# End of attention in an attention + two-MoE kernel: own PSUM banks for the last group, a softplus without reciprocal, first expert weights split between groups

## What is computed

```python
# 1. attention: each token is a mix of itself and its 6 predecessors, per head
w = softmax(weight_gen, axis=-1)                     # (B, S, 8 heads, 7 taps)
out = einsum('bshk,bskhg->bshg', w, x_unfolded)      # x_unfolded: 7 shifted rows
# 2. first mixture of experts (8 experts, 2 choices a token)
logits = x @ w_gate
noise_scale = log1p(exp(x @ w_noise))                # softplus
noisy = logits + noise_scale * noise
top2, top2_w = two largest of noisy, softmax over the two
out[mask] += top2_w * (relu(x[mask] @ w1[e]) @ w2[e])
# 3. second mixture (8 experts, 1 choice), by cosine to expert_emb over tau
logits = normalized(x) @ normalized(expert_emb).T / tau
out[mask] = gate_w * (relu(x[mask] @ w1[e]) @ w2[e])
```

## Time and profile before

| | us |
|---|---|
| median of 3 runs (1231.30, 1233.33, 1233.25) | 1233.25 |
| the profiled execution | 1230.78 |
| its span, first to last instruction | 1229.0 |
| outside the span | 1.78 |
| attention, up to the end of the last row sum | 120.2 |
| logits of the last group copied | 126.6 |
| first mixture's PE stream begins | 206.4 |

### The profile page before, as it was taken

How to read it: one execution, slowest core, us unless ns; L and a number is a source line. 1 busy time by engine, 2 the same in 40 slices (tenths; PEclk the granted TensorE clock), 3 DMA queues, 4 the chain that set the end, 5 groups by cost and what they waited for, 6 DMA issues and landing times.

```text
span 1229.0 us, 27241 instructions
## 1 busy us (share of the span) xinstructions
PE 1098.7 (89%) x8062; PEld 1041.1 (85%) x8062; DVE 753.6 (61%) x1412; ACT 548.3 (45%) x1543; POOL 523.5 (43%) x635
## 2 busy tenths in 40 slices
PE   1999168999999999999999999787289999999997
PEld 0566056999999999999999999766279999999997
DVE  8998896546465554646545464476854654466663
ACT  2112266445454544545445454356644554455552
POOL 5878102444444444444444444400324444444444
PEclk9999589999999999999999999989589999999999
DMA  9111200313122131312213111173712313124511
GB/s 330 67 58 65 60 1 21 95 42 95 38 73 67 41 102 42 94 38 79 64 41 97 39 37 38 40 257 104 239 50 72 100 39 102 40 61 128 141 56 36
DMA packets 51188, 97.89 MB, mean 80 GB/s; under 512 B 9651, under 2 KB 33051, under 8 KB 50876
## 3 DMA queue, kind: packets, MB, share of 16 engines
q1 hardware_dynamic: 33084, 61.77, 16.4%
q0 software_dynamic: 18048, 35.42, 9.9%
HBM read 69.62 MB, written 29.10 MB: 80 GB/s over the span
## 4 chain that ended last, share of the span: by engine, by line
PE 78%; DVE 13%; issue 3%; POOL 2%; ACT 2%; DMA 2%; DVEq 0%; POOLq 0%; ACTq 0%; SPq 0%
PE banks L605 22%; PE banks L607 11%; PE banks L591 9%; PE banks L597 7%; PE banks L596 7%; PE banks L592 7%; PE banks L593 7%; DVE prods L856 3%; PE banks L567 2%; POOL prods L415 2%; PE banks L575 2%; PE banks L576 2%; PE banks L529 1%; DVE choices L1064 1%; PE banks L519 1%
## 5 line engine op out<-in xcount | busy, mean ns | idle before, releaser
L1014 DVE SCALAR_TENSOR_TENSOR h_lo<-banks,h_hi 128x256 fp32r<-128x256 f32 x736 | 312.0, 424 | 373.6 <-ACT h_hi L743 319.0
L743 ACT ACTIVATE h_hi<-banks 128x256 fp32r<-128x256 f32 x736 | 282.5, 384 | 450.8 <-PE banks L597 340.1
L605 PE MATMUL banks<-w_hl,h_hi 128*128 128x384 f32 x1472 | 466.4, 353 | 0.0
L607 PE MATMUL banks<-w_hl,h_lo 128*128 128x192 f32 x1472 | 371.1, 252 | 0.0
L607 PEld LDWEIGHTS banks<-w_hl,h_lo 128*128 128x128 f32 x1472 | 279.6, 190 | 0.0
L605 PEld LDWEIGHTS banks<-w_hl,h_hi 128*128 128x128 f32 x1472 | 276.0, 188 | 0.2
L430 POOL DMA_INDIRECT x_slots<-token_rows,gather_idx x192 | 192.3, 1002 | 107.2 <-POOL gather_idx L427 76.8
L591 PE MATMUL banks<-x_hi_a,w_hi 128*128 (+1 forms) x736 | 224.9, 306 | 1.7 <-DVE x_hl_b L982 1.7
L592 PE MATMUL banks<-x_hi_a,w_lo 128*128 (+1 forms) x736 | 206.6, 281 | 0.0
L597 PE MATMUL banks<-x_hl_b,w_lo 128*128 (+1 forms) x736 | 206.3, 280 | 0.0
L596 PE MATMUL banks<-x_hl_b,w_hi 128*128 (+1 forms) x736 | 205.8, 280 | 0.0
(11 more groups left out here) (172 smaller groups left out, 1271.7 us busy)
## 6 DMA issues: line engine op xcount, KB each, us to landing
raw<-in_moe_w SPq DMA_DIRECT2D x17, 768.0 KB
choices<-choice_rows SPq DMA_DIRECT2D x28, 384.0 KB, 3.8
raw<-in_moe_w SPq DMA_DIRECT2D x17, 512.0 KB
raw<-in_moe_w SPq DMA_DIRECT2D x34, 256.0 KB
x_halo<-in_x SPq DMA_DIRECT2D x2, 2688.0 KB, 15.0
token_rows<-stage SPq DMA_DIRECT2D x14, 384.0 KB, 2.3
token_rows<-rows SPq DMA_DIRECT2D x14, 384.0 KB, 3.9
x_slots<-token_rows,gather_idx POOLq DMA_INDIRECT x192
```

Source lines behind the costliest of these rows:

```text
L605: mm(y[:, i, 0:2 * D], h_hi[:, c % HBUFS, t], w2_hl[u][:, c, :, :], start=c == 0, stop=False)
L607: ins = mm(y[:, i, 0:D], h_lo[:, c % HBUFS, t], w2_hl[u][:, c, 0, :], start=False, stop=c == FC - 1)
L743: sc.activation(h_hi[:, c % HBUFS, :], banks[:, c % HBANKS, 0:BLOCK], ACT.Relu).then_inc(h_hi_ready[m], 1)
L1014: v.scalar_tensor_tensor(h_lo[:, c % HBUFS, :], banks[:, c % HBANKS, 0:BLOCK], 0.0, h_hi[:, c % HBUFS, :].bitcast(F32), ALU.max, ALU.subtr ...
```

## The change

Four things are done. **(a)** The last group (g = 13) gets banks 6 and 7 for its transposes, bank 5 for its logits and `prods[0][:, 0]` in place of `rows_t`; its transposes stand ahead of the logits of group 12 and no longer wait for any logits. The ten idle matmuls go, and the probe that loads the Exp table stands an iteration earlier on ACT, ahead of `take_turned(0, 12)`. **(b)** Softplus: ACT itself computes |z| and exp(-|z|) (u), DVE computes w = 1 + u, then (w - 1) - u and max(z, 0) minus that, while ACT takes ln(w), and DVE adds the two. Reciprocal, tie handling and the products are gone. **(c)** The first expert's weights are split in eight pieces (four of w1, 128x512, and four of w2, 128x384): ACT makes the high parts in iterations 2 to 9 of the attention loop, behind `take_turned`; POOL makes the low parts in iterations 4 to 11, ahead of the pair additions. **(d)** DVE scales the embeddings in iteration 6 of the attention loop, behind `finish_rows(5)`, not after the last group.

```diff
@@ -27,6 +27,8 @@
 HALVES = BLOCK // P
 GROUP = 4
 CHOICE_BUFS = 3
+HI_FROM, LO_FROM = 2, 4
+EMB_AT = 6
 TURN_AT = 2
 Y_AT = 1
 X_SPLIT_AT = 4
@@ -189,6 +191,7 @@
         raw_in = sem("raw_in")
         weights_ready = sem("weights_ready")
         weight_hi = sem("weight_hi")
+        first_hi = sem("first_hi")
         emb_sumsq = sem("emb_sumsq")
         emb_scaled = sem("emb_scaled")
         emb_t = sem("emb_t")
@@ -270,15 +273,28 @@
                     body(end, 1 - u, expert + 1, u)
             finish(ends[E - 1] - 1)
 
-        def turned_bank(m, u):
-
-            return 4 - 2 * u * m
-
-        def logits_bank(m):
-
-            return 4 + 2 * m
+        def turned_bank(m, g, u):
+
+            return 6 if m == 0 and g == NG - 1 else 4 - 2 * u * m
+
+        def logits_bank(m, g):
+
+            if m == 0:
+                return 5 if g == NG - 1 else 4
+            return 6
+
+        def turned_rows(m, g):
+
+            return prods[0][:, 0].rearrange("p (i c) -> p i c", c=P) if m == 0 and g == NG - 1 else rows_t[:]
 
         row_table = (row_no, signed_row[:].rearrange("p b j -> p (b j)"))
+
+        def weight_part(c):
+
+            half = FC // 2
+            if c < half:
+                return slice(c * F // half, (c + 1) * F // half), None
+            return None, slice(2 * (c - half), 2 * (c - half) + 2)
 
         def parity(eng, g):
             return g % 2 if isinstance(g, int) else eng.snap(g % 2)
@@ -395,6 +411,13 @@
                     allow_small_or_imprecise_dtypes=True).then_inc(consts_ready, 1)
 
 
+            def first_lo(c):
+
+                w1_part, w2_part = weight_part(c)
+                if w1_part is not None:
+                    return gp.tensor_tensor(w1_lo[0][:, :, w1_part], raw1[:, :, w1_part], w1_hi[0][:, :, w1_part].bitcast(F32), ALU.subtract)
+                return gp.tensor_tensor(w2_hl[0][:, w2_part, 1, :], raw2[:, w2_part, :], w2_hl[0][:, w2_part, 0, :].bitcast(F32), ALU.subtract)
+
             per_tap = lambda a: a.unsqueeze(2).to_broadcast([P, J * H, K])
             for b in range(1, B):
                 pool.wait_ge(tap_max, b + 1)
@@ -406,6 +429,11 @@
 
 
             for g in range(NG):
+                if 0 <= g - LO_FROM < FC:
+                    pool.wait_ge(first_hi, g - LO_FROM + 1)
+                    ins = first_lo(g - LO_FROM)
+                    if g - LO_FROM == FC - 1:
+                        ins.then_inc(weights_ready, 1)
                 taps = prods[g % 2]
                 for to, other in PAIRS:
                     if other < FIRST:
@@ -414,13 +442,6 @@
                         pool.wait_ge(second_prods, g + 1)
                     gp.tensor_tensor(taps[:, to], taps[:, to], taps[:, other], ALU.add).then_inc(taps_added, 1)
 
-
-            pool.wait_ge(raw_in, 64)
-            gp.tensor_copy(w1_hi[0][:], raw1[:]).then_inc(pool_step, 1)
-            gp.tensor_copy(w2_hl[0][:, :, 0, :], raw2[:]).then_inc(pool_step, 1)
-            pool.wait_ge(pool_step, 2)
-            gp.tensor_tensor(w1_lo[0][:], raw1[:], w1_hi[0][:].bitcast(F32), ALU.subtract)
-            gp.tensor_tensor(w2_hl[0][:, :, 1, :], raw2[:], w2_hl[0][:, :, 0, :].bitcast(F32), ALU.subtract).then_inc(weights_ready, 1)
 
             def mixture(m, to, limit, written):
                 def gather(n):
@@ -502,21 +523,21 @@
             def turn_rows(m, g, u, tiles):
 
                 pe.wait_ge(rows_ready[m], g + 1)
-                if m == 0 and g > 0:
+                if m == 0 and 0 < g < NG - 1:
                     pe.wait_ge(logits_ready[0], g)
                 for i in range(GROUP // 2):
                     pair = tiles[:, 2 * i:2 * i + 2, :].rearrange("p i (f r) -> p r (i f)", r=THIRDS)
                     for r in range(THIRDS):
                         bank, at = divmod(i * THIRDS + r, 4)
-                        ins = nc.tensor.transpose(banks[:, turned_bank(m, u) + bank, at * P:(at + 1) * P], pair[:, r, :], ident[:])
+                        ins = nc.tensor.transpose(banks[:, turned_bank(m, g, u) + bank, at * P:(at + 1) * P], pair[:, r, :], ident[:])
                 ins.then_inc(rows_turned[m], 1)
 
             def group_logits(m, g, right, width):
                 pe.wait_ge(rows_t_ready[m], g + 1)
                 for i in range(GROUP // 2):
-                    to = banks[:, logits_bank(m), i * 2 * width:(i + 1) * 2 * width]
+                    to = banks[:, logits_bank(m, g), i * 2 * width:(i + 1) * 2 * width]
                     for r in range(THIRDS):
-                        ins = mm(to, rows_t[:, i * THIRDS + r, :], right[:, r, :], start=r == 0, stop=r == THIRDS - 1)
+                        ins = mm(to, turned_rows(m, g)[:, i * THIRDS + r, :], right[:, r, :], start=r == 0, stop=r == THIRDS - 1)
                 ins.then_inc(logits_done[m], 1)
 
             def sum_products(g, inner=None):
@@ -541,10 +562,8 @@
             for g in range(2, NG):
                 sum_products(g, lambda: group_logits(0, g - 2, *router))
                 turn_rows(0, g - 1, (g - 1) % 2, stage[(g - 1) % 2])
-            keep_clock(5)
+            turn_rows(0, NG - 1, 1, stage[1])
             group_logits(0, NG - 2, *router)
-            turn_rows(0, NG - 1, 1, stage[1])
-            keep_clock(5)
             group_logits(0, NG - 1, *router)
 
             pe.wait_ge(emb_scaled, 1)
@@ -661,14 +680,14 @@
 
             def take_turned(m, g, u=0):
                 act.wait_ge(rows_turned[m], g + 1)
-                turned = banks[:, turned_bank(m, u):turned_bank(m, u) + 2, :]
-                sc.copy(rows_t[:].rearrange("p i c -> p (i c)"),
+                turned = banks[:, turned_bank(m, g, u):turned_bank(m, g, u) + 2, :]
+                sc.copy(turned_rows(m, g).rearrange("p i c -> p (i c)"),
                         turned.rearrange("p k c -> p (k c)")[:, 0:GROUP // 2 * THIRDS * P]).then_inc(rows_t_ready[m], 1)
 
             def take_logits(m, g, width):
                 act.wait_ge(logits_done[m], g + 1)
                 sc.copy(logits[:, bass.ds(g * GROUP, GROUP), 0:width],
-                        banks[:, logits_bank(m), 0:GROUP * width].rearrange("p (i e) -> p i e", i=GROUP)).then_inc(logits_ready[m], 1)
+                        banks[:, logits_bank(m, g), 0:GROUP * width].rearrange("p (i e) -> p i e", i=GROUP)).then_inc(logits_ready[m], 1)
 
             def take_weights(g):
                 b, jj = divmod(g, GB)
@@ -690,6 +709,13 @@
             act.wait_ge(act_step, 1)
             sc.sqrt(emb_norm[0:E, 1:2], emb_norm[0:E, 0:1]).then_inc(emb_sumsq, 1)
 
+            def first_weights_hi(c):
+
+                w1_part, w2_part = weight_part(c)
+                if w1_part is not None:
+                    return sc.copy(w1_hi[0][:, :, w1_part], raw1[:, :, w1_part])
+                return sc.copy(w2_hl[0][:, w2_part, 0, :], raw2[:, w2_part, :])
+
             take_weights(0)
             take_weights(1)
             take_weights(2)
@@ -698,10 +724,15 @@
                 if g + 1 < NG:
                     take_weights(g + 1)
                 take_logits(0, g - 2, 2 * E)
+                if g == NG - 1:
+                    sc.activation(table_probe[:], ident[:, 0:1], ACT.Exp)
                 take_turned(0, g - 1)
+                if 0 <= g - HI_FROM < FC:
+                    if g == HI_FROM:
+                        act.wait_ge(raw_in, 64)
+                    first_weights_hi(g - HI_FROM).then_inc(first_hi, 1)
+            take_turned(0, NG - 1)
             take_logits(0, NG - 2, 2 * E)
-            sc.activation(table_probe[:], ident[:, 0:1], ACT.Exp)
-            take_turned(0, NG - 1)
             take_logits(0, NG - 1, 2 * E)
 
             def mixture(m):
@@ -764,11 +795,13 @@
                     ins.then_inc(hi_rows_ready[m], 1)
 
             def softplus_exp():
+                act.wait_ge(logits_ready[0], NG)
+                sc.activation(r["soft_u"][:], logits[:, :, E:2 * E], ACT.Abs).then_inc(act_step, 1)
+                act.wait_ge(act_step, 2)
+                sc.activation(r["soft_u"][:], r["soft_u"][:], ACT.Exp, scale=-1.0).then_inc(route_act[0], 1)
                 act.wait_ge(route_ask[0], 1)
-                sc.activation(r["soft_u"][:], r["soft_u"][:], ACT.Exp, scale=-1.0).then_inc(route_act[0], 1)
+                sc.activation(r["soft_ln"][:], r["soft_w"][:], ACT.Ln).then_inc(route_act[0], 1)
                 act.wait_ge(route_ask[0], 2)
-                sc.activation(r["soft_ln"][:], r["soft_w"][:], ACT.Ln).then_inc(route_act[0], 1)
-                act.wait_ge(route_ask[0], 3)
                 sc.activation(gate[1][:], gate[1][:], ACT.Exp).then_inc(route_act[0], 1)
 
             softplus_exp()
@@ -865,6 +898,12 @@
                                 banks[:, 2 * u:2 * u + 2, 0:GHALF].rearrange("p h (i d) -> p h i d", d=D),
                                 prods[u][:, LAST].rearrange("p (h i d) -> p h i d", h=2, d=D), ALU.add).then_inc(rows_ready[0], 1)
 
+            def scale_embeddings():
+                dve.wait_ge(emb_sumsq, 1)
```

(27 more changed lines are left out.)

## The result

| | before | after |
|---|---|---|
| median, us (6 runs each) | 1232.24 | 1225.11 (1223.56 to 1226.43) |
| ratio of the runs | | 0.9945, 95% interval 0.9934 to 0.9955 |
| the profiled execution, us | 1230.78 | 1223.82 |
| its span, us | 1229.0 | 1222.1 |
| end of the last row sum | 120.24 | 122.71 |

The kernel is faster by 0.55% (0.45% to 0.66%), some 6.8 us (the two medians lie 7.1 apart); the forecast was 8.4. The span lost 6.9 us, of which 6.5 are there when DVE multiplies with the noise.

What follows compares the result with a forecast made beforehand. The prediction took the unbranched string behind the last row sum, and DVE in the attention loop, as the bounds. Terms: -2.2 - 6.6 + 0.4 = -8.4 us, from 1233.25 to 1224.8 us; range 1222.0 to 1228.4.

Steps and rivals of the forecast that it cites:

- Part a: Last row sum to last logits' copy: own banks end the copy at 124.42 instead of 126.58, gain 2.2 us.
- the two sets of logits: Tail behind the last group's transposes: PE needs 1.42 + 1.54 us for two sets of twelve matmuls.
- Part b: Softplus, logits' copy to noise multiplication: 10.36 us becomes 3.78, gain 6.6 us, bounds 6.0 and 6.8.
- rivals 2 and 3: Softplus tables: |z| needs two more loads, 1227.4 us, chance 0.03; Ln begins 1.4 later, 1226.2 us, chance 0.03.
- Part c: Attention loop: sixteen weight pieces fit POOL's 1.45 us and ACT's 0.59 us of room; cost 0, bounds 0 and 0.5.
- Part d: Attention loop, iteration 6: scaling gets in between POOL's second and third additions; loss 0.4 us, bounds 0.3 and 2.2.
- The asking time of 67.15: Iteration 6: the embeddings' multiplication on DVE asks 1.23 us after the row sum's start at 65.92.
- the price of losing: Iteration 6: if the multiplication lets POOL's third addition pass, the next products start at 69.1, 2.1 to 2.2 late.
- rival 1: Iteration 6: the embeddings' multiplication loses its place to POOL's third addition; 1.8 us more, 1226.6 us, chance 0.22.
- The sum: Whole kernel: -2.2 - 6.6 + 0.4 = -8.4 us, giving 1222.4 from the profiled execution and 1224.8 from the median.
- Rival 5: PE clock at L567, behind the tail: gain given back by 1 or 2 us either way; not carrying through, chance 0.03.
- Rival 4: Attention loop: holes give no cover, pieces paid 13.0 us, 1237.9 us; chance 0.03, a third to two thirds 0.06.

Runs made afterwards that it cites:

- e2: Changed kernel with the first weights' pieces out of the loop, GpSimd splitting them behind it again; 1227.64 us, ratio 0.9969.
- e5: Changed kernel with the norm's addition and reciprocal moved to iteration 5, so the embeddings' multiplication asks earlier; 1223.38 us, one execution.
- e7: Changed kernel with the norm's addition and reciprocal in iteration 5 and the embeddings' multiplication ahead of iteration 6's row sum; 1226.08 us, one execution.
- e1: Changed kernel with the embeddings scaled behind the last group again, not in the loop; 1223.32 us, ratio 0.9928.
- e8: Changed kernel with the embeddings scaled behind the last group and two low parts in each of iterations 8 to 11; 1223.83 us, one execution.
- e3: Changed kernel with |z|, reciprocal, tie handling and products of the softplus on VectorE again; 1231.80 us, ratio 0.9994.
- e4: Changed kernel with one rows buffer, banks 4 and 5, idle matmuls and table probe at their old places; 1227.32 us, ratio 0.9959.
- e10: Changed kernel with the embeddings scaled in iteration 9 instead of 6; 1224.23 us, one execution.
- e6: Changed kernel with the embeddings scaled behind the last group and 16 idle matmuls ahead of the row tables; 1221.49 us, ratio 0.9917.
- e9: Changed kernel with the embeddings scaled behind the last group and 26 idle matmuls ahead of the row tables; 1221.78 us, ratio 0.9921.

## Why the prediction came out as it did

- **Part a** (2.2, bounds 1.7 and 2.5): 6.34 us from the last row sum to the last copy before, 3.86 after: 2.48. The term that was put too long is the two sets of logits, 1.42 + 1.54; in one stream the 24 matmuls took 2.61. The clock stayed at 1.00 in the tail (116 to 127 us) and the probe was hidden, as written: the copy behind it starts 0.63 us after the start of the last row sum, as it did before.
- **Part b** (6.6): 10.36 to 3.86 us, 6.50, where 3.78 was worked out for the new chain. |z| needed no table of its own, and Ln began 0.01 behind the load (129.09 after 127.80 + 1.28), which speaks against rivals 2 and 3. The split of the gain was right too: without POOL's lock the old softplus takes 9.16 us, and the rest belongs to the reciprocal and its company.
- **Part c** (0): right, by the room worked out. POOL's hole left 0.20 us where 0.15 was worked out, and ACT's piece, 0.62, fitted ahead of the copy of tap weights; no period with a piece alone grew. What the prediction missed is what part c is for: it put the 1.2 us of the lock down to part b, while without part c the addition of 1 meets the same lock, sooner by what part a gains, and loses 2.25 us (e2).
- **Part d** (a loss of 0.4, bounds 0.3 and 2.2): this is the step that failed. The multiplication was to get in ahead of GpSimd's third addition and had to let it pass, in 1.98 us instead of about 0.25. "I take a loss of 0.4 us, since the only such meeting in the trace went that way" rested on a wait that had begun 4 us before the boundary, and the one at hand began 0.09 before it. The asking time of 67.15 and the price of losing, 69.1, were right to 0.1 us; e5 and e7 show that asking 0.4 us ahead is enough to win. The loop lost 2.03 us by that, and another 0.40 in the next period that nothing in the prediction foresaw and no run explains. The prediction had written this case down as rival 1, at 0.22, and a period of 9 us as its sign.
- **The sum.** 2.48 + 6.50 - 2.47 = 6.51 at the multiplication with the noise. The remaining 0.4 of the span's 6.9 lies in the row tables (0.1) and the mixtures (0.3), under the differences between profiled executions. The measured 6.8 (5.5 to 8.1) contains rival 1's 6.6 and not quite the forecast's 8.4. That the time of 1224.8 came out so close is luck: it was anchored at a median of 1233.25, where three more runs gave 1232.24 for all six. From there the same sum gives 1223.8, and the measured 1225.1 is 1.3 over it, as the profiled execution is 1.4 over its own forecast of 1222.4.
- **Rival 5** leaves a trace too: the clock at the row tables rises in the second window in the changed kernel as before (0.94 and 0.90), so nothing was given back there; a late rise, as in e1, would have cost 0.6 us.
- **Rival 4** was rightly small, but its mechanism is real: e8 calls it up with two pieces where one fits, and it costs 2.2 us for 2 x 1.05 + 2 x 0.5 of overshoot, less the ring's room.

## What to carry to other kernels

A small instruction on the engine that bounds a loop is not costed by its length but by what it must wait for: 0.3 us of work on VectorE cost 2.0 beside GpSimd's additions, and nothing behind the loop, where its engine waits anyway. What one part of a change is worth can hang on another: GpSimd's tail cost 1.2 us in the kernel before and costs 2.25 in e2, where part a has brought the instructions that it holds forward. And work put into the holes of an engine is free only up to the hole; e8 shows the bill 0.5 to 1.05 us beyond it.

## What was not expected of the hardware

- A VectorE instruction that needs the shared ports gets them at the next boundary between GpSimd's instructions if it asks 0.4 us or more ahead (ends 0.1 us behind the boundary), and waits for one whole instruction more if it asks 0.08 to 0.09 us ahead (1.98 us instead of 0.3, in the changed kernel and likewise in e2, e3, e4 and e10). The Trainium skill ("SBUF — State Buffer", "Who interferes with whom") has issue order decide; the runs agree with that if the next GpSimd instruction counts as issued somewhat before its recorded start. Where between 0.09 and 0.4 us the line lies was not tried.
- Two microseconds of idle TensorE behind 16 idle matmuls let the clock fall to 0.59 in the window from 154 to 156 us (e6), though it had risen only in the window from 150 to 152 us (0.76), with 1.00 in the one between; with work all through (e9) it stayed at 1.00. In the attention loop a hole of 2.25 us let it fall to 0.50 in e3 (76 to 78 us) and one of 2.28 us left it at 1.00 in the changed kernel, so the length of the hole alone doesn't decide.
